# Attention masks from bucket numbers in HBM, in a kernel of attention and two expert layers on one core

## What is computed

```
q_bits = (einsum('bhsd,dk->bhsk', q, proj) > 0)
k_bits = (einsum('bhsd,dk->bhsk', k, proj) > 0)
powers = 2 ** arange(6)
q_bucket = sum(q_bits * powers, axis=-1)
k_bucket = sum(k_bits * powers, axis=-1)
mask   = q_bucket[:, :, :, None] == k_bucket[:, :, None, :]
scores = where(mask, scale * (q @ k^T), -1e9)
attn   = softmax(scores);  out = attn @ v
x = moe(out)        # x @ w_in, relu, square, affine, @ w_out
y = moe2(x)         # routed: the best of 8 experts for each token
```

## Time and profile before

| | |
|---|---|
| median of 3 runs | 749.17 us |
| the profiled execution | 748.38 us |
| its span, first to last instruction | 746.6 us |
| TensorE busy | 703.5 us, 94% |
| VectorE busy | 423.2 us, 57% |
| ScalarE busy | 321.9 us, 43% |
| GpSimd busy | 264.5 us, 35% |
| granted clock of TensorE, mean | 0.98 of full |
| start, to the first scores | 0 to 36.4 us |
| the 8 pairs | 36.4 to about 268 us |
| first expert layer, routing, second expert layer | from about 268 us |

### The profile page before, as it was taken

The page is one execution under the profiler, slowest core; times in us unless marked ns, Lnnn a source line. Parts: engine busy times, 40 slices in busy tenths (PEclk is TensorE's granted clock), DMA queues, the critical chain, the costliest instruction groups (busy, mean ns, idle before and its releaser), DMA issues.

```text
span 746.6 us, 12026 instructions
## 1 busy us (share of the span) xinstructions
PE 703.5 (94%) x3809; PEld 591.6 (79%) x3809; DVE 423.2 (57%) x795; ACT 321.9 (43%) x634; POOL 264.5 (35%) x269
## 2 busy tenths in 40 slices
PE   5889999999999999999999999999964999999995
PEld 2469999999999887888888888888863788778884
DVE  0399999999999855458345645643346411331110
ACT  0078878878878842222211222221414322442221
POOL 1646777677677740035006203500001112112121
PEclk9999999999999999999999999999986999999998
DMA  9822311321341110003001100010117611101010
GB/s 277 259 64 56 106 53 53 99 59 53 95 121 56 57 57 1 0 2 113 0 1 56 56 0 0 1 58 0 57 59 252 254 57 36 50 29 58 28 58 33
DMA packets 22348, 50.80 MB, mean 68 GB/s; under 512 B 3136, under 2 KB 5312, under 8 KB 22304
## 3 DMA queue, kind: packets, MB, share of 16 engines
q1 hardware_dynamic: 19008, 42.34, 18.1%
q0 software_dynamic: 2320, 7.34, 3.0%
q10 hardware_dynamic: 976, 0.56, 0.4%
HBM read 43.95 MB, written 6.55 MB: 68 GB/s over the span
## 4 chain that ended last, share of the span: by engine, by line
PE 87%; DVE 4%; DMA 4%; SPq 2%; issue 1%; ACT 1%; ACTq 0%; POOL 0%; POOLq 0%; DVEq 0%
PE ps L1191 9%; PE ps L1210 8%; PE ps L1355 6%; PE ps L1356 6%; PE ps L1357 6%; PE ps L1337 6%; PE ps L1338 6%; PE ps L1339 6%; PE ps L1224 5%; PE ps L1225 4%; PE ps L1466 3%; PE ps L1468 3%; PE ps L1467 3%; PE ps L1426 3%; PE ps L1428 3%; PE ps L1427 3%
## 5 line engine op out<-in xcount | busy, mean ns | idle before, releaser
L677 ACT ACTIVATE relu<-ps 128x512 f32<-128x512 f32 x48 | 28.7, 598 | 190.6 <-PE ps L1339 190.6
L833 DVE TENSOR_TENSOR pt_lo<-ps,pt_hi 128x384 fp32r<-128x384 f32 x192 | 100.2, 552 | 10.2 <-ACT pt_hi L624 6.3
L624 ACT ACTIVATE pt_hi<-ps 128x384 fp32r<-128x384 f32 x192 | 87.8, 498 | 40.6 <-PE ps L1210 25.5
L613 ACT ACTIVATE probs<-ps,neg_max 128x768 f32<-128x768 f32 x96 | 87.2, 908 | 30.6 <-DVE neg_max L824 30.4
L1210 PE MATMUL ps<-cst,probs 128*128 128x128 f32 x576 | 90.3, 274 | 1.1 <-DVE pt_lo L833 1.0
L824 DVE TENSOR_REDUCE neg_max<-ps 128x1 f32<-128x768 f32 x96 | 90.9, 948 | 0.0
L1355 PE MATMUL ps<-wo_hi,g_hi 128*128 128x512 f32 x192 | 76.1, 396 | 0.6 <-DVE xt_lo L901 0.6
L1356 PE MATMUL ps<-wo_lo,g_hi 128*128 128x512 f32 x192 | 75.5, 393 | 0.0
L1357 PE MATMUL ps<-wo_hi,g_lo 128*128 128x512 f32 x192 | 75.3, 392 | 0.0
L1337 PE MATMUL ps<-xt_hi,wi_hi 128*128 128x512 f32 x192 | 75.1, 391 | 0.0
L1210 PEld LDWEIGHTS ps<-cst,probs 128*128 128x128 f32 x576 | 70.0, 144 | 6.3 <-DVE pt_lo L833 2.1
(11 more groups left out here) (156 smaller groups left out, 1505.6 us busy)
## 6 DMA issues: line engine op xcount, KB each, us to landing
w_raw<-w SPq DMA_DIRECT2D x16, 512.0 KB, 6.3
raw_k<-kT SPq DMA_DIRECT2D x32, 192.0 KB, 3.4
raw_q<-qT SPq DMA_DIRECT2D x32, 192.0 KB, 3.7
wi_raw<-w_in SPq DMA_DIRECT2D x4, 1024.0 KB, 5.0
wo_raw<-w_out SPq DMA_DIRECT2D x4, 1024.0 KB, 5.3
pair_raw<-qT SPq DMA_DIRECT2D x8, 384.0 KB, 8.9
pair_raw<-kT SPq DMA_DIRECT2D x8, 384.0 KB, 14.9
raw_v<-v SPq DMA_DIRECT2D x16, 192.0 KB, 2.4
```

The source lines that it names most:

```text
L833: nc.vector.tensor_tensor(pt_lo[c % 2][sl], unit(tt, h).rearrange("p (k q) -> p k q", k=3), pt_hi[c % 2][sl].bitcast(F32), ALU.subtract).t ...
```

## The change

The bucket numbers themselves are computed once, in the start, and kept in HBM as bf16 (`buckets`). For a pair, SP loads the numbers of both heads, for q and k, each row of numbers repeated over 64 partitions (`bucket_of`, 128 x 1536), a pair ahead. VectorE compares them with the partition's own bucket (`lane`) in one instruction of 128 x 1536 at tile 4 (`MASK_TILE`), which gives both masks, for q and for k, as 0 and 1. The six mask products of TensorE and the six comparisons of VectorE in a pair go. GpSimd, which copied the masks before, now scales the one for q by 2^60 and subtracts 1 from the one for k, so that the product is again 0 or -2^60; the second of these is a two-input instruction.

```diff
-MASK_TILES = (2, 3, 5, 6, 8, 9)
-MASK_UNITS = len(MASK_TILES)
+MASK_UNITS = 6
+MASK_TILE = 4
+ID_ROWS = 32
...
+            sp.wait_ge(ids_kept, 2)
+            for a in range(3):
+                sp.dma_start(buckets[:, :, MASK_W * a:MASK_W * (a + 1)],
+                             bucket_ids[ID_ROWS * a:ID_ROWS * a + NH, :, :]).then_inc(ids_out, 16)
+            sp.wait_ge(ids_out, 48)
+
+            def load_buckets(i):
+
+                sp.wait_ge(masks_staged, i + (MASK_UNITS - 1))
+                for z in range(2):
+                    sp.dma_start(bucket_of[half(z, True), :, :], buckets[ds(i * 2 + z, 1), :, :].to_broadcast(
+                        [HD, 2, SEQ])).then_inc(ids_in, 16)
+
             with sp.Fori(1, PAIRS) as i:
+                load_buckets(i)
                 load_heads(i, False)
...
-                pool.wait_ge(masks_staged, i * MASK_UNITS + MASK_UNITS)
+                pool.wait_ge(masks_staged, i + MASK_UNITS)
                 pool.wait_ge(scores_done, i * TILES_PER_PAIR + (QT * (z + 1) - TILES_PER_PAIR))
                 m = half(z, True)
-                for c, stack in ((0, qb), (1, kb)):
-                    copied(stack[z][m, :], mask_st[m, c, :], 1.0, masks_in, i * 4 + (2 * z + c + 1))
+                copied(qb[z][m, :], mask_st[m, 0, :], BIG, masks_in, i * 4 + (2 * z + 1))
+                hold()
+                G.tensor_tensor(kb[z][m, :], mask_st[m, 1, :], ones_c[m, 0:1].to_broadcast([HD, SEQ]),
+                                ALU.subtract).then_inc(masks_in, 1)
+                pool.wait_ge(masks_in, i * 4 + (2 * z + 2))
...
                 v_.wait_ge(scores_done, i * TILES_PER_PAIR + (tt + 1))
-                if tt in MASK_TILES and not last:
-
+                if tt == MASK_TILE and not last:
+
+                    v_.wait_ge(ids_in, i * 32 + 32)
                     v_.wait_ge(masks_in, i * 4 + 4)
-                    m = MASK_TILES.index(tt)
-                    stage_mask(m, slice(0, P), mask_st[:, m // 3, :], beside(z, MASK_W)).then_inc(masks_staged, 1)
+                    nc.vector.tensor_scalar(mask_st[:, :, :], bucket_of[:, :, :], lane[:, :], None,
+                                            ALU.is_equal).then_inc(masks_staged, 1)
...
+            prepare(nc.vector.memset(powers[:, :], 0.0), 1)
+            prepare(nc.vector.tensor_tensor(weighed, heads, iota128[0:NH * NBITS, 0:HD].unsqueeze(1).to_broadcast(
+                [NH * NBITS, NH, HD]), ALU.mult), 2)
+            weights = x_rows[0:NH * NBITS, 2, 0, 0:NH]
+            prepare(nc.vector.tensor_reduce(weights, weighed, AX, ALU.add), 3)
+            prepare(nc.vector.tensor_copy(powers[:, 0:NH], weights), 4)
+            prepare(nc.vector.tensor_scalar(lane_hi[:, :], tokid[:, 0:1], float(HD), -float(HD), ALU.is_gt, ALU.mult), 5)
+            prepare(nc.vector.scalar_tensor_tensor(lane[:, :], tokid[:, 0:1], -1.0, lane_hi[:, :], ALU.add, ALU.add), 6)
+
+            def keep_ids(c):
+                v_.wait_ge(ids_turned, c + 1)
+                nc.vector.tensor_scalar(bucket_ids[:, c, :], ps[0:3 * ID_ROWS, 7 - c, 256:512], 1.0 / 32, None,
+                                        ALU.mult).then_inc(ids_kept, 1)
...
                 for m in units:
                     keep_bits(m)
+                keep_ids(c)
...
                 for m in range(3 * c, 3 * c + 3):
                     pe.wait_ge(bits_done, m + 1)
-                    masks(0, m, first_mask(m)).then_inc(masks_turned, 1)
+                    masks(m, first_mask(m)).then_inc(masks_turned, 1)
+                pe.wait_ge(prepared, 4)
+                for a in range(3):
+                    last_mm = mm(ps[ID_ROWS * a:ID_ROWS * (a + 1), 7 - c, 256:512], powers[:, :],
+                                 bits[:, c, MASK_W * a:MASK_W * (a + 1)], start=True, stop=True)
+                last_mm.then_inc(ids_turned, 1)
...
-                if tt in MASK_TILES and not last:
-                    last_mm = masks(i + 1, MASK_TILES.index(tt), beside(tt % 2, MASK_W))
...
             pe.wait_ge(masks_staged, MASK_UNITS)
+            pe.wait_ge(ids_kept, 2)
             pair(0, True, False)
```

More of the change, by code:

```diff
@@ L67, in program @@
     y_rows = nc.dram_tensor("y_rows", (TOK, DM), F32).ap()
+    buckets = nc.dram_tensor("buckets", (NH, 2, SEQ), BF16).ap()
     with ExitStack() as ctx:
@@ L125, in program @@
         mask_st = sb("mask_st", [P, 2, SEQ], BF16, 2)
+        bucket_of = sb("bucket_of", [P, 2, SEQ], BF16, 2)
+        bucket_ids = sb("bucket_ids", [3 * ID_ROWS, 2, MASK_W], BF16, 2)
+        powers = sb("powers", [NH * NBITS, ID_ROWS], BF16, 2)
+        lane_hi = sb("lane_hi", [P, 1], F32)
+        lane = sb("lane", [P, 1], F32)
         raw_q = [sb(f"raw_q{z}", [P, SEQ], F32) for z in range(2)]
@@ L263, in program @@
         masks_staged = sem("masks_staged")
+        prepared = sem("prepared")
+        ids_turned = sem("ids_turned")
+        ids_kept = sem("ids_kept")
+        ids_out = sem("ids_out")
+        ids_in = sem("ids_in")
         masks_in = sem("masks_in")
@@ L798, in keep_bits, with first_mask_of @@
                                         ALU.is_gt).then_inc(bits_done, 1)
-            def stage_mask(m, part, dst, src):
+            def first_mask_of(m, part, dst, src):
                 col = MASK_W * (m % 3)
@@ L876, in pair, with prepare @@
                             invert(i - 1, c + CHUNKS_PER_PAIR)
+            def prepare(ins, count):
+                ins.then_inc(prepared, 1)
+                v_.wait_ge(prepared, count)
+            heads = patt[:, :].rearrange("p (h b) -> p h b", b=HD)
+            weighed = x_rows[0:NH * NBITS, 0:2, :, :].rearrange("p a t d -> p (a t d)")[:, 0:NH * HD].rearrange(
+                "p (h b) -> p h b", b=HD)
+            prepare(nc.vector.memset(powers[:, :], 0.0), 1)
[10 more added lines that the diff above has]
+                                        ALU.mult).then_inc(ids_kept, 1)
             for c, stack in ((0, qb), (1, kb)):
@@ L885, in _ @@
                         v_.wait_ge(masks_turned, m + 1)
-                        placed = stage_mask(m, half(z, True), stack[z], first_mask(m))
+                        placed = first_mask_of(m, half(z, True), stack[z], first_mask(m))
                         if z == 1:
@@ L1138, in _, with masks @@
             mm = nc.tensor.matmul
-            def masks(i, m, dst):
-                return mm(dst, patt[:, ds(i * P, P)],
+            def masks(m, dst):
+                return mm(dst, patt[:, 0:P],
                           bits[:, m // 3, MASK_W * (m % 3):MASK_W * (m % 3) + MASK_W], start=True, stop=True)
@@ L1150, in first_masks @@
                     pe.wait_ge(masks_staged, 2)
+                    pe.wait_ge(ids_kept, 1)
                 for m in range(3 * c, 3 * c + 3):
                     pe.wait_ge(bits_done, m + 1)
-                    masks(0, m, first_mask(m)).then_inc(masks_turned, 1)
+                    masks(m, first_mask(m)).then_inc(masks_turned, 1)
[4 more added lines that the diff above has]
+                last_mm.then_inc(ids_turned, 1)
             pe.wait_ge(projb_in, 16)
@@ L1175, in turn_back, with scores @@
                 return last_mm
-            def scores(i, tt, first, last):
+            def scores(i, tt, first):
                 z, j = divmod(tt, QT)
@@ L1239, in pair @@
                     if tt < TILES_PER_PAIR - 2:
-                        scores(i, tt + 2, first, last_)
+                        scores(i, tt + 2, first)
                     elif not last_:
-                        scores(i + 1, tt + 2 - TILES_PER_PAIR, False, False)
+                        scores(i + 1, tt + 2 - TILES_PER_PAIR, False)
                     c, part = divmod(tt - 4, CHUNK_TILES)
@@ L1258, in pair @@
                         turn_xt(1)
-            scores(0, 0, True, False)
-            scores(0, 1, True, False)
+            scores(0, 0, True)
+            scores(0, 1, True)
             pe.wait_ge(masks_staged, MASK_UNITS)
+            pe.wait_ge(ids_kept, 2)
             pair(0, True, False)
```

## The result

The changed kernel takes 755.04 us (median of 5 runs, 753.34 to 756.73) against 748.96 (5 runs, 747.22 to 749.23) of the kernel before on the same chip: a ratio of 1.0088, 95% interval 1.007 to 1.0106, so 6.1 us slower by the medians, 5.2 to 7.9 by the interval. The profiled execution took 756.73 with a span of 754.9, which is 8.3 more than the span before.

The account below looks back on a forecast made before the run. TensorE was taken to bound the kernel (87% of the span). Gains of 2.6 us in pairs 1 to 6 and 0.7 in pair 0, less 1.4 at the start, gave 1.9 less: 749.17 to 747.3 us, 8 in 10 within 745.4 to 753.2.

Parts of the forecast that it names:

- it slips into the gap between the two, with 0.2 us to spare: Loop, tile 4: VectorE's comparison, asked at 156.92, fits between GpSimd's two subtractions of head 1's split (156.96, 157.13).
- x: Loop: how much earlier GpSimd is if its mask instruction for k is cheaper than 1.83 us.
- the forecast case: Loop: the comparison runs between GpSimd's two subtractions without waiting; 746 to 748.3 us in all, chance 0.42.
- The rival: Loop: the comparison waits out GpSimd's running subtraction; 0.9 us lost a pair at x = 1.0, 752.9 us; chance 0.22.
- The half-way case: Loop: each caught pair gives GpSimd the time that lets the next through; 752.5 us instead of 757.8.
- The loop without the wait: Pairs 1 to 6: six mask products gone give 0.48 us a pair, less 0.05 for small waits; 2.6 gained.
- The comparison: VectorE, 1536 columns ahead of tile 4's maximum: 0.56 us, bounds 0.43 to 1.75; costs nothing in the loop at 0.56.
- GpSimd's masks for head 0: Loop: they end at 173.50, before tile 0 of the next pair needs them at 173.73; 0.1 to 0.2 us left.
- Pair 0: VectorE is on the chain there; its comparisons and TensorE's products gone, less the wide comparison: 0.7 us of 0.9 counted.
- The start: Additions before the first scores: 1.05 us for k's numbers, 0.35 mid-projections; 1.4 lost, bounds 0.4 to 2.3.
- The loads of the numbers: SP's store and loads of bucket numbers in the start cost nothing; 1 to 3 us if transfers take 2 more.
- The chances: Whole kernel: faster 0.40, same 0.31, slower 0.29, from chances given to the forecast and its rivals.

Follow-up runs that it names:

- run 3: The changed kernel with one more 64-column GpSimd instruction, result unused, between the mask rows and head 1's split: 747.68 us, ratio 0.9976 to the kernel before.
- run 2: The changed kernel with a one-input instead of a two-input GpSimd instruction for the mask rows of k: 752.01 us, ratio 1.0026 to the kernel before.
- run 1: The changed kernel with the comparison ahead of tile 5's maximum instead of tile 4's: 747.44 us, ratio 0.9964 to the kernel before.
- run 5: As run 1, with the start's added VectorE and TensorE instructions moved to where those engines wait anyway: 744.42 us, ratio 0.9929 to the kernel before.
- run 6: As run 5, with the one-input GpSimd instruction of run 2 for the mask rows of k: 745.05 us, ratio 0.9953 to the kernel before.
- run 4: The kernel before with only the changed kernel's start and store to HBM, numbers not read back, loop masks as before: 751.3 us, ratio 1.0024.
- run 7: The changed kernel, comparison at tile 4, in the form that also writes a sum, which is unused: 755.6 us, ratio 1.0102 to the kernel before.

## Why the prediction was wrong

The mechanism was seen, priced and given the wrong chance. Point by point:

- **The failed step**: "it slips into the gap between the two, with 0.2 us to spare". The prediction put GpSimd's second subtraction at 157.13 and the request at 156.92. The first of these rested on GpSimd's mask instruction for k at 1.83 us, "the row of the same width". It took 1.46, x = 0.37 in the prediction's letters. The margin of 0.21 became -0.15 (162.42 against 162.57), and -0.08 to -0.17 over the six pairs, so the rest of that reckoning was right within 0.1. Run 3 puts 0.44 us back and gets the forecast case (0.26 us to spare). The step was thus wrong in size, by 0.37 us in an estimate bounded at 0.83 to 1.83, but behind so small a margin stood a wait of 1.5.
- **The rival's working held.** It took the wait to be the time to the subtraction's end, and so it nearly is: 1.83 - 0.15 = 1.68 to the end, 0.43 more for the rest, 2.11 in all. The row of the cast on which the rival was built had shown the same, an end 0.28 behind GpSimd's. Both rows put the end of the wait 0.15 to 0.18 ahead of the end of GpSimd's row (the cast alone takes 0.43, the comparison 0.61), so the prediction's prices were a little high. A wait of 1.50, of which 0.08 hides, costs 29.32 - 27.90 = 1.42 a pair. The half-way case, in which a caught pair lets the next one through, did not come: all six wait, since GpSimd's round starts behind `split_v`, which waits for TensorE (`[1.46 <-PE ps L1281]` above), so it shifts with the loss and the phase stays. At x = 1.0 the rival gave 0.9 a pair; run 2, with x = 1.0 in fact, lost 28.63 - 27.90 = 0.73 a pair.
- **The loop without the wait**: 27.90 us a pair against 27.8, a gain of 0.37 for the 0.43 counted. Tiles at 2.06 and 2.27 for 2.05 and 2.25. Right.
- **The comparison**: 0.61 for 0.56. Right by choosing the cast's bytes per us. The estimate from the Trainium skill, VectorE: DVE Perf Modes, "The perf-mode tier table", had been the same 0.56; the trace is 0.05 above it.
- **GpSimd's masks for head 0**: no wait of TensorE for them in runs 1, 5 and 6. Right; run 6 shows that even 0.63 less is worth nothing.
- **Pair 0**: 0.7 us of gain. TensorE's scores of tiles 4 and 10 in pair 0 say it: of the kernel before, of run 5, and of the changed kernel.

```profile
43.36 0.62 PE L1191 MATMUL ps<-ka,qa 128*128 128x512 f32 x2
...
56.51 0.51 PE L1191 MATMUL ps<-ka,qa 128*128 128x512 f32 x2
```

```profile
42.96 0.62 PE L1257 MATMUL ps<-ka,qa 128*128 128x512 f32 x2
...
55.63 0.58 PE L1257 MATMUL ps<-ka,qa 128*128 128x512 f32 x2
```

```profile
46.45 0.71 PE L1249 MATMUL ps<-ka,qa 128*128 128x512 f32 x2
...
58.91 0.58 PE L1249 MATMUL ps<-ka,qa 128*128 128x512 f32 x2
```

Run 5 is 0.20 early in tile 0 (36.18 for 36.38) and 0.88 early in tile 10: 0.7. Right, with the comparison at tile 5; in the changed kernel itself the clock hides it.

- **The start**: 1.4 us lost. To the first scores it was 1.17, with 0.15 in the middle (0.35 counted) and 1.03 for the numbers of k (1.05 counted). The 1.03 is firm. The 0.15 is not: with the same start the bits of k came between 33.41 (run 3) and 34.59 (run 4), against 33.85 before, and which it is depends on how VectorE's new product and GpSimd's subtraction meet. **A second step failed here**: what the prediction did not have is the clock behind it. By the rows above, the changed kernel is 3.09 late in tile 4, 1.9 us more than in tile 0, and 2.40 in tile 10, since pair 0 gives its 0.7 back. Run 1 against run 5, the same instructions at either clock, gives 2.1 from tile 0 to tile 4. A term for TensorE's clock behind a longer wait ahead of the first scores was missing altogether.
- **The loads of the numbers**: no wait of VectorE in pair 0, whose comparison starts at 47.84 straight behind the instruction before it. Right.
- **The chances**: the parts give 0.32 for no change (0.23 + 0.09) and 0.28 for slower (0.22 + 0.06), where the prediction has 0.31 and 0.29. Nothing hangs on it.

The sum with measured terms: loop +6.3 for -2.6, start and pair 0 +2.5 for +0.7, and the rest of the program -0.5: 8.3 us, the difference of the spans. The medians differ by 6.1. The 2.2 between them is less than what the rest of the program varies by from trace to trace (476.5 to 480.8); what makes it vary stays open, since a profile shows one execution. Run 1 shows it too: its profiled start and pair 0 lost 2.8 and six pairs gained 2.2, yet its median is 2.7 us below that of the kernel before.

## What to carry to other kernels

Two engines that lock each other out make the time a step function of their phase: price the step first. Then ask how far each uncertain duration ahead of it would have to be off to cross it, and give the crossing a chance by that, not by where the best guess falls. Here an error of 0.21 us in one estimated GpSimd instruction was enough for 8.5 us (6 x 1.42). An instruction that waits for another engine in this way belongs where that engine is idle for certain (in the loop, a tile later, it was), not in a gap of 0.2 us. And work added where TensorE waits may cost more than its own time: look at the granted clock behind it.

## What the runs showed of the hardware

- A GpSimd two-input instruction of 64 x 768 took 1.46 us with a bf16 input and a broadcast second one, 1.83 with two full float32 inputs; the one-input form took 0.83 from bf16 and from float32 alike.
- The wait between the engines goes both ways and hides in the duration of the instruction, not in idle time: VectorE 2.11 for 0.61, GpSimd 2.05 for 1.83 in run 3. GpSimd's side need not be a two-input instruction (pair 0 of run 1: 1.05 for 0.61), and VectorE's can be one (run 4: 2.81 for 1.28). In the start of the changed kernel GpSimd's subtraction took 2.57 for 1.80, beside VectorE's new two-input product:

```profile
20.66 1.41 DVE L917 TENSOR_TENSOR x_rows<-patt,cst 96x1024 f32<-96x1024 bf16 x1
...
21.18 2.57 POOL L515 TENSOR_TENSOR kb<-raw_k,ka 64x768 fp32r<-64x768 f32 x1 [0.18 <-POOL qa L511]
```

- The comparison that also writes a sum costs three times the plain one (1.81 for 0.61) and did not wait for GpSimd in any of its six rows in the loop.
- In the profiled executions with 1.9 us of TensorE idle time ahead of the first scores (the changed kernel, runs 1 to 4 and 7), the granted clock from 36 to 47 us was 0.53 to 0.69; in those with 0.9 to 1.1 (the kernel before, runs 5 and 6) it was 1.00. Each is one execution, and no run changed the idle time alone. The length of a wait by itself does not decide it either: ahead of tile 2's scores TensorE stood idle for 1.82 us in the kernel before and for 2.04 in run 5, and the clock stayed at 1.00. In pair 0 of run 7, on the other hand, a wait of 1.56 us was followed by 0.50 again. What sets the clock back in the one case and not in the other stays open. The two rows of the waits that did not, kernel before first:

```profile
39.83 0.59 PE L1191 MATMUL ps<-ka,qa 128*128 128x512 f32 x2 [1.82 <-ACT probs L613]
```

```profile
39.86 0.58 PE L1257 MATMUL ps<-ka,qa 128*128 128x512 f32 x2 [2.04 <-ACT probs L642]
```
